# A fused dynamic convolution and MLP: all matmuls of the loop as 64-row tiles on the two row halves, with the transposes inside a second product

## What is computed

```python
# x: (4, 4096, 192); weight_gen: (4, 4096, 8, 7); w_in: (192, 2048); w_out: (2048, 192)
w = exp(weight_gen - max(weight_gen, -1)); w = w / (sum(w, -1) + 1e-9)
out[b,s,h,g] = sum_k w[b,s,h,k] * x_padded[b, s+k, h, g]     # 7 taps, 8 heads of 24 channels
h = out.reshape(16384, 192) @ w_in
y = (s * relu(h)**2 + b) @ w_out                              # (16384, 192), float32
```

## Time and profile before

| | |
|---|---|
| Median of 3 runs | 1248.54 us (1246.58 to 1249.45) |
| The profiled execution | 1249.54 us, span in the trace 1247.7 us |
| Mean granted TensorE clock | 0.991 of full speed |
| PE busy | 96% of the span, 7392 matmuls and as many weight loads |
| DVE, ACT, POOL busy | 80%, 63%, 14% |
| Chain that ended last | PE 73%, ACT 10%, DVE 9%, issue 7% |

### The profile page before, as it was taken

One profiled execution on the slowest core, in us unless ns is written; L12 is line 12 of the kernel. 1 busy time (PEld: TensorE's weight loads), 2 busy tenths in 40 slices (PEclk: granted clock), 3 DMA queues, 4 the chain that ended last, 5 costly groups with the idle time before them and its releaser, 6 DMA issues.

```text
span 1247.7 us, 20056 instructions
## 1 busy us (share of the span) xinstructions
PE 1203.6 (96%) x7392; PEld 1030.6 (83%) x7392; DVE 995.4 (80%) x1162; ACT 780.2 (63%) x844; POOL 172.8 (14%) x97
## 2 busy tenths in 40 slices
PE   3899999999999999999999999999999999999998
PEld 3788888888888888888888888888888888888887
DVE  7887778887778887779887779877788877788853
ACT  3466666666665666665666566666566666666664
POOL 7311011111011110011110111110111110111100
PEclk8899999999999999999999999999999999999999
DMA  5111101111101111101111101111001111011000
GB/s 171 36 49 36 48 16 44 48 48 35 48 13 48 48 48 35 48 13 48 48 48 35 38 22 48 48 39 44 21 39 48 48 35 48 14 47 48 13 0 26
DMA packets 18404, 50.98 MB, mean 41 GB/s; under 512 B 2140, under 2 KB 9563, under 8 KB 18394
## 3 DMA queue, kind: packets, MB, share of 16 engines
q1 hardware_dynamic: 18245, 50.27, 11.9%
q10 hardware_dynamic: 149, 0.59, 0.2%
HBM read 38.27 MB, written 12.58 MB: 41 GB/s over the span
## 4 chain that ended last, share of the span: by engine, by line
PE 73%; ACT 10%; DVE 9%; issue 7%; POOL 1%; DVEq 0%; DMA 0%; ACTq 0%; POOLq 0%
PE op L661 26%; PE hp L637 22%; PE op L663 11%; PE hp L648 11%; ACT r L386 5%; ACT r L390 5%; DVE tap L492 2%; DVE acc L507 2%; PE hp L622 2%; DVE g_hi L534 2%; DVE attn_b L512 1%; PE hp L625 1%; DMA x_in<-in_x 0%; POOL tap_pool L318 0%; POOL acc L327 0%
## 5 line engine op out<-in xcount | busy, mean ns | idle before, releaser
L661 PE MATMUL op<-wo,g_hi 128*128 128x384 f32 x2048 | 608.9, 367 | 2.3 <-DVE g_lo L538 2.3
L663 PE MATMUL op<-wo,g_lo 128*128 128x192 f32 x2048 | 513.4, 251 | 0.0
L386 ACT ACTIVATE r<-hp 128x1024 f32<-128x1024 f32 x256 | 260.1, 1016 | 401.6 <-PE hp L648 397.1
L538 DVE TENSOR_TENSOR g_lo<-r,g_hi 128x1024 fp32r<-128x1024 f32 x256 | 360.0, 1406 | 80.9 <-ACT g_hi L397 76.4
L661 PEld LDWEIGHTS op<-wo,g_hi 128*128 128x128 f32 x2048 | 386.0, 188 | 37.3 <-issue 26.7
L663 PEld LDWEIGHTS op<-wo,g_lo 128*128 128x128 f32 x2048 | 392.7, 192 | 0.0
L637 PE MATMUL hp<-xT,w_hi 128*128 128x512 f32 x1024 | 322.8, 396 | 3.7 <-ACT r L386 1.9
L390 ACT ACTIVATE r<-r 128x1024 f32<-128x1024 f32 x256 | 271.5, 1061 | 7.9
L492 DVE TENSOR_TENSOR tap<-x_in,w_soft 128x768 f32<-128x768 f32 (+1 forms) x192 | 232.8, 1226 | 0.1
L637 PEld LDWEIGHTS hp<-xT,w_hi 128*128 128x128 f32 x1024 | 183.6, 189 | 38.1 <-DVE xT L520 2.2
L637 PE MATMUL hp<-xT,w_lo 128*128 128x512 f32 x512 | 203.4, 397 | 0.0
(11 more groups left out here) (46 smaller groups left out, 418.6 us busy)
## 6 DMA issues: line engine op xcount, KB each, us to landing
x_in<-in_x SPq DMA_DIRECT2D x30, 960.0 KB, 4.8
out<-out_sb SPq DMA_DIRECT2D x31, 384.0 KB, 2.3
w_in<-in_weight_gen SPq DMA_DIRECT2D x32, 112.0 KB, 2.0
wo_raw<-in_moe_w_out SPq DMA_DIRECT2D x4, 384.0 KB, 7.0
w_raw<-in_moe_w_in SPq DMA_DIRECT2D x4, 256.0 KB, 5.4
x_in<-in_x SPq DMA_DIRECT2D x1, 768.0 KB, 6.8
x_in<-in_x ACTq DMA_DIRECT2D x1, 540.0 KB
w_raw<-in_moe_w_in SPq DMA_DIRECT2D x8, 64.0 KB, 4.8
```

The lines of the kernel that those rows point to most:

```text
L386: nc.scalar.activation(r[:, b, :], hp[:, PAIR * b:PAIR * (b + 1), :], ACT.Relu).then_inc(relu_done, 1)
L538: nc.vector.tensor_tensor(g_lo[:, buf, tiles, :], pair, g_hi[:, buf, tiles, :].bitcast(F32), ALU.subtract).then_inc(g_lo_ready, 1)
L661: nc.tensor.matmul(op[:, t, 0:2 * D], g_hi[:, g % 2, j, cols], wo[:, k, :, :].rearrange("p a d -> p (a d)"), start=(k == 0), stop=False)
L663: mm = nc.tensor.matmul(op[:, t, 0:D], g_lo[:, g % 2, j, cols], wo[:, k, 0, :], start=False, stop=(k == FT - 1))
```

## The change

Every matmul with 128 rows in the loop becomes two with 64 rows, one on each half of the partitions. Two matmuls that run side by side write different banks, so each bank is written by one half first and by the other half later; the semaphores `h_bank_left` and `op_bank_left` keep the halves apart. The first product has 18 pairs of matmuls of 512 columns per group; `h_ready` of the even pair comes with pair 15 of them, that of the odd pair with the last. The passes with `xT2` now follow the passes with `xT1` bank by bank, so group 0 needs the copies in the upper partitions (`t_hi_up_ready`, `t_lo_up_ready`) after three pairs. The second product goes by pairs of token tiles outside and hidden tiles j inside, so that pair 2g + 1 is waited for after two units of work. The transposes are 64-row tiles too: 8 for `attn_a` into banks 0 and 1 after a quarter of the second product of group 2, 4 for `attn_b` into banks 2 and 3 after its second quarter. On ScalarE, relu of pair 7 and `hi_of_attn` now stand ahead of the square and the high part of pair 6. `hp` is read for the copies across two banks. In the last step the output is finished in two halves of 2 token tiles instead of 3 and 1.

```diff
+        def block_a():
+            return hp[:, 0:2, 0:STEP * D2].rearrange("p h (t c) -> p t h c", t=STEP)
@@ ScalarE, step
                 for q in range(PAIRS - 1):
                     relu(i, q, first)
+                    if q == PAIRS - 2:
+                        relu(i, PAIRS - 1, first)
+                        if not last:
+                            hi_of_attn(i + 1)
                     square(i, q)
...
-                relu(i, PAIRS - 1, first)
-                if not last:
-                    hi_of_attn(i + 1)
@@ TensorE
+            def transpose_attn_a():
                 for t in range(STEP):
-                    last = nc.tensor.transpose(hp[:, 0, t * P:(t + 1) * P], attn_a[:, t, :], ident[:, :])
+                    for h in range(2):
+                        last = nc.tensor.transpose(hp[:, h, t * D2:(t + 1) * D2], attn_a[rows[h], t, :], ident[rows[h], rows[h]])
...
+            FIRST_BANKS = [((0, True), (2, True), (1, False), (3, False)),
+                           ((1, True), (3, True), (0, False), (2, False))]
...
+                for n, both in enumerate(zip(passes_of(0), passes_of(1))):
+                    if n == 0 and not (first and g == 0):
+                        pe.wait_ge(relu_done, i * PAIRS + 2 * g - 1)
+                    if n == 6 and not (first and g == 0):
+                        pe.wait_ge(relu_done, i * PAIRS + 2 * g)
+                    if n == 3 and g == 0:
+                        pe.wait_ge(t_hi_up_ready, i + 1)
+                        pe.wait_ge(t_lo_up_ready, i + 1)
+                    if n in (12, 15):
+                        pe.wait_ge(h_bank_left, left + n // 3 - 3)
+                    for j, w, xt, start, stop in both:
+                        mm = nc.tensor.matmul(hp[:, j, :], w, xt, start=start, stop=stop)
+                    if n in (5, 11):
+                        mm.then_inc(h_bank_left, 1)
+                    if n in (14, 17):
+                        mm.then_inc(h_ready, 1)
+
+            def second_product(i, g, first=False, last=False, transposes_next=False):
...
+                for n in range(STEP):
+                    transposes_here = transposes_next and n < 2
+                    tiles = ((0, 1), (2, 3), (1, 0), (3, 2))[n]
+                    if n >= PAIR:
+                        pe.wait_ge(op_bank_left, 2 * n_before + n - 1)
+                    for j in range(GROUP):
+                        if n == 0 and j % PAIR == 0:
+                            pe.wait_ge(g_lo_ready, i * PAIRS + 2 * g + j // PAIR + 1)
+                        k = g * GROUP + j
+                        for h, t in enumerate(tiles):
+                            nc.tensor.matmul(op[:, t, 0:2 * D], g_hi[rows[h], g % 2, j, t * P:(t + 1) * P], ...)
+                        if transposes_here and j == GROUP - 1:
+                            if n == 0:
+                                pe.wait_ge(sum_ready, (K - 1) * (i + 2))
+                            pe.wait_ge(relu_done, (i + 1) * PAIRS + n - 1)
+                        for h, t in enumerate(tiles):
+                            mm = nc.tensor.matmul(op[:, t, 0:D], g_lo[rows[h], g % 2, j, t * P:(t + 1) * P], ...)
+                    if n < PAIR:
+                        mm.then_inc(op_bank_left, 1)
+                    if transposes_here and n == 0:
+                        transpose_attn_a()
+                    if transposes_here and n == 1:
+                        transpose_attn_b()
```

More of the change, by code:

```diff
@@ L159, in mix_and_mlp @@
         g_used = sem("g_used")
+        h_bank_left = sem("h_bank_left")
+        op_bank_left = sem("op_bank_left")
         out_sums_ready = sem("out_sums_ready")
@@ L225, in store_last @@
             def store_last():
-                first = (STEPS - 1) * STEP * row
-                for n, (a, b) in enumerate(((0, EARLY), (EARLY, STEP))):
+                last_rows = out_rows[:, (STEPS - 1) * STEP * row:STEPS * STEP * row].rearrange("p (t d) -> p t d", t=STEP)
+                for n in range(2):
                     sp.wait_ge(last_output_ready, n + 1)
-                    sp.dma_start(out_rows[:, first + a * row:first + b * row],
-                                 out_sb[:, a:b, :].rearrange("p t d -> p (t d)")).then_inc(last_stored, FETCH)
+                    sp.dma_start(last_rows[:, n * PAIR:(n + 1) * PAIR, :], out_sb[:, n * PAIR:(n + 1) * PAIR, :]).then_inc(last_stored, FETCH)
             load_w(0)
@@ L544, in last_output @@
                 dve.wait_ge(out_stored, FETCH * (STEPS - 1))
-                for n, tiles in enumerate((slice(0, EARLY), slice(EARLY, STEP))):
+                for n in range(2):
                     if n == 0:
@@ L549, in last_output @@
                         dve.wait_ge(g_used, NG * STEPS)
-                    m = tiles.stop - tiles.start
-                    nc.vector.scalar_tensor_tensor(out=out_sums[:, tiles, 0:D], in0=op[:, tiles, 0:D], scalar=s_col[:, 0:1],
-                                                   in1=bias[:, :].unsqueeze(1).to_broadcast([P, m, D]),
+                    nc.vector.scalar_tensor_tensor(out=out_sums[:, n * PAIR:(n + 1) * PAIR, 0:D], in0=op[:, n * PAIR:(n + 1) * PAIR, 0:D], scalar=s_col[:, 0:1],
+                                                   in1=bias[:, :].unsqueeze(1).to_broadcast([P, STEP // 2, D]),
                                                    op0=ALU.mult, op1=ALU.add).then_inc(last_part_ready, 1)
                     dve.wait_ge(last_part_ready, n + 1)
-                    nc.vector.scalar_tensor_tensor(out=out_sb[:, tiles, :], in0=op[:, tiles, D:2 * D], scalar=s_col[:, 0:1],
-                                                   in1=out_sums[:, tiles, 0:D], op0=ALU.mult,
+                    nc.vector.scalar_tensor_tensor(out=out_sb[:, n * PAIR:(n + 1) * PAIR, :], in0=op[:, n * PAIR:(n + 1) * PAIR, D:2 * D], scalar=s_col[:, 0:1],
+                                                   in1=out_sums[:, n * PAIR:(n + 1) * PAIR, 0:D], op0=ALU.mult,
                                                    op1=ALU.add).then_inc(last_output_ready, 1)
@@ L624, in transpose_attn @@
                 for u in range(STEP // 2):
-                    last = nc.tensor.transpose(hp[:, 1, u * P:(u + 1) * P],
-                                               attn_b[:, 2 * u:2 * u + 2, :].rearrange("p t d -> p (t d)"), ident[:, :])
+                    for h in range(2):
+                        last = nc.tensor.transpose(hp[:, 2 + h, u * D2:(u + 1) * D2],
+                                                   attn_b[rows[h], 2 * u:2 * u + 2, :].rearrange("p t d -> p (t d)"),
+                                                   ident[rows[h], rows[h]])
@@ L627, in transpose_attn @@
                 last.then_inc(t_ready, 1)
+            FIRST_BANKS = [((0, True), (2, True), (1, False), (3, False)),
+                           ((1, True), (3, True), (0, False), (2, False))]
             def first_product(i, g, first=False):
[L630 to L666, removed]
+                def passes_of(h):
+                    for j, own in FIRST_BANKS[h]:
+                        f = slice((g * GROUP + j) * P, (g * GROUP + j + 1) * P)
+                        f2 = slice((g * PAIR + j // 2) * P, (g * PAIR + j // 2 + 1) * P)
+                        some = [(w1_hi[rows[h], f], xT1[rows[h], 0, :]), (w1_hi[rows[h], f], xT1[rows[h], 1, :]),
+                                (w1_lo[rows[h], f], xT1[rows[h], 0, :])]
+                        if own:
+                            some += [(w2_hi[rows[h], f2], xT2[rows[h], 0, :]), (w2_hi[rows[h], f2], xT2[rows[h], 1, :]),
+                                     (w2_lo[rows[h], f2], xT2[rows[h], 0, :])]
+                        for n, (w, xt) in enumerate(some):
+                            yield j, w, xt, own and n == 0, not own and n == len(some) - 1
@@ new lines, in first_product @@
+                left = 2 * (i * NG + g)
+                for n, both in enumerate(zip(passes_of(0), passes_of(1))):
[14 more added lines that the diff above has]
+                        mm.then_inc(h_ready, 1)
@@ new lines, in second_product @@
+            def second_product(i, g, first=False, last=False, transposes_next=False):
+                n_before = i * NG + g
+                if first:
+                    pe.wait_ge(wo_lo_ready, g + 1)
+                if not (first and g == 0):
+                    pe.wait_ge(g_used, n_before)
+                for n in range(STEP):
[8 more added lines that the diff above has]
+                        for h, t in enumerate(tiles):
+                            nc.tensor.matmul(op[:, t, 0:2 * D], g_hi[rows[h], g % 2, j, t * P:(t + 1) * P],
+                                             wo[rows[h], k, :, :].rearrange("p a d -> p (a d)"),
+                                             start=(k == 0 and n < PAIR), stop=False)
+                        if transposes_here and j == GROUP - 1:
[3 more added lines that the diff above has]
+                        for h, t in enumerate(tiles):
```

(12 more changed lines are left out.)

17 lines of the change are left out of this document (10 added, 7 removed).

## The result

| | before | after |
|---|---|---|
| Median (lowest to highest) | 1247.66 us (1246.58 to 1249.45) | 1273.87 us (1271.76 to 1274.46) |
| Profiled execution, span | 1249.54, 1247.7 us | 1271.76, 1269.8 us |
| Mean granted clock | 0.991 | 0.980 |
| Matmuls | 7392 | 13216 |

The ratio is 1.0206 [1.0187, 1.0224]: the change makes the kernel 26 us slower, where 22 us less was forecast. 1273.87 is near rival 1's lower price, 1276.

A forecast was written before the change was run, and what follows sets the result against it. TensorE's own stream was taken to set the time, busy 37.17 of 37.70 us per step. From 1249.54, 30 steps by -0.8, first step +1.0, last +0.7 gave 1227 profiled, 1226 us median; range 1205 to 1365.

The forecast's parts named there:

- rival 1: GpSimd's request precedes VectorE's cast of pair 1: TensorE waits 2.68 us, 1276 us total, 1360 with clock falls; chance 0.38.
- Where it hangs: Whether GpSimd's addition or VectorE's cast of pair 1 asks first; sum put GpSimd 0.13 us ahead, forecast took the cast.
- the forecast's order: VectorE's cast of pair 1 goes ahead of GpSimd's first addition; TensorE then waits 1.03 us for pair 1.
- What goes: On TensorE, shape changes (0.36 per group, 1.44 us per step) and the 0.5 hole before transposes vanish: 1.9 to 2.0.
- The doubled matmuls: TensorE's 64-row matmuls cost nothing extra per column: 0.232 per pair, 0.287 per unit; six transposes keep 0.66 per step.
- rival 3: TensorE's sequencer limits the unit to 0.40: +5.7 us per step, 1430 us; chance 0.06.
- rival 4: TensorE's units get a little slower, 0.30 each, and eat the gain: 37.7 per step, no change; chance 0.07.
- Pair 7: Second product of group 3: TensorE waits 0.18 us for g_lo of pair 7.
- Pair 1: Second product of group 0: TensorE waits 1.03 us for g_lo of pair 1, or 2.68 if GpSimd asks first.
- The clock's price: A 2.68 wait every step may bring 5.7 us at half clock each time, 2.8 lost: 1276 becomes 1360 us.
- The two ends: First step +1.0 us and last step +0.7 us, outside the 30 steps in between.
- 12.89: VectorE's way from g_lo of pair 6 to g_lo of pair 1, taken as 12.89 us of unbroken work.

The follow-up runs named there:

- experiment 2: Changed kernel, but GpSimd starts its additions only when g_lo of pair 0 of the next step is done; 1212.87 us, ratio 0.9721.
- experiment 1: Changed kernel, but GpSimd starts its additions only when g_lo of pair 1 of the next step is done; 1193.88 us, ratio 0.957.
- experiment 3: Changed kernel, but each second product waits for its odd pair after eight units again, GpSimd left as it is; 1209.05 us, ratio 0.9685.
- experiment 5: Changed kernel with the odd pair awaited after eight units and GpSimd adding after g_lo of pair 1; 1179.99 us, ratio 0.946.
- experiment 7: As experiment 5, but relu of pair 7 and hi_of_attn go back behind the high part of pair 6 on ScalarE; 1218.49 us, ratio 0.9766.

## Why the prediction was wrong

**The step that failed is "Where it hangs".** In the kernel before, GpSimd asks 0.70 us behind the start of the cast. The working put its request 0.13 ahead of the cast; the changed kernel has it 0.19 ahead. The prediction then set the sum aside, "TensorE's side has more terms that can only grow", and took the other case. That sentence held an asymmetry that no row showed, and the terms shrank. In the step shown above T, the start of the second product of group 2, is 640.87; its rows:
```profile
640.87 0.34 PE L693 MATMUL op<-wo,g_hi 64*128 64x384 f32 x2
...
647.64 1.23 DVE L546 TENSOR_TENSOR g_lo<-r,g_hi 128x1024 fp32r<-128x1024 f32 x1 [0.77 <-ACT g_hi L403]
...
649.79 1.03 ACT L392 ACTIVATE r<-hp 128x1024 f32<-128x1024 f32 x1 [0.95 <-PE hp L671]
```
On GpSimd's side, T to the next step is 5.17 instead of 5.25, from there to relu 0 it is 3.75 as taken, and from relu 0 to GpSimd 6.92 instead of 6.99: T + 15.84 instead of 15.99. On VectorE's side, `g_lo` of pair 6 starts at T + 6.77 instead of 6.86 and the cast follows 9.26 later as taken: T + 16.03 instead of 16.12. So the sum was right to 0.06 us. What followed from the order was nearly right on both sides: with the requests in the forecast's order (experiment 2) a step is 36.53 (36.9 forecast) and the time 1212.87 us (1226 forecast); with GpSimd first it is 38.15 (38.56 in rival 1). Experiments 1 and 3 show the two parts of the wait, GpSimd's blocks and TensorE's early need, each taken away alone.

**What goes** was right. No 0.36 per group is left in the changed kernel, and the hole of 0.53 ahead of the transposes is gone; a wait of 0.16 of the weight loads is left (experiment 5's list of waits). Experiment 5 makes the gain visible where nothing waits: 37.70 - 35.49 = 2.2 per step.

**The doubled matmuls** cost nothing per column, as taken: pairs 0.231, units 0.287 (15 from 672.15 to 676.45), with eight instructions in a unit. This closes rivals 3 and 4. (Rival 3's price had a slip: 0.40 - 0.287 is 0.113 and not 0.12, so 5.2 per step and not 5.7.) The transposes came out just under their lower bound of 0.33: eight occupy 0.21 and four 0.08 to 0.09, twelve 0.30 instead of 0.66. What is left of the block from T to the next step, 5.17 - 4.59 - 0.30 = 0.28, is the wait for the sums and small restarts.

**Pair 7** waits less than the 0.18 computed: the third unit of that second product starts at 650.79, 0.04 late.

**Pair 1** waits 2.45, computed 2.68: the first block is 1.65 and not 1.7, the second 1.5 and not 1.65. Step by step at full clock: 38.56 less 0.08 (transposes' block), 0.07 (pairs), 0.08 (group 3) and 0.23 (pair 1) is 38.10; 38.15 is measured.

**The clock's price** was the badly sized term of rival 1. The same idle stretch in every step dropped it in 9 of 28 steps, not in none or all, and a fall cost 39.73 - 38.15 = 1.58, not 2.8: the fall shown above lasted some 3.4 us (from about 663.7 to 667.1), where the first step of the earlier trace rows had stood at 0.50 for over 5.7. Idle stretches of 0.68, 0.74 and 0.98 in every step (experiments 2, 3 and 7) brought no fall. What makes one stretch of 2.31 bring a fall and the next not, no run shows.

**The two ends** were taken at +1.7 together; by the account above everything outside the 28 steps gave back 4.9 us, since the first of GpSimd's additions came 2.15 earlier, the second step and the last but one ran in the forecast's order, and the last waits only 0.27 and 0.95 (1.8 had been taken).

**Chances.** Rival 1 was given 0.38 against 0.44 for the forecast. The sum that was written down spoke for rival 1, and the blind margin, 0.13 against 27 slots and waits, did not justify turning it over: the two should at best have been even, with the time put by the sum.

The Trainium skill (SBUF — State Buffer, section "Who interferes with whom") states "Issue order, not op shape, decides who blocks." Experiment 2, the second step and the last but one of the changed kernel agree, with 0.49 to 0.68 us of idle on TensorE in one order and 2.31 in the other.

**The two steps with the other order** can be read in part. They are written out on VectorE, while the 28 between run inside its loop (`dve.Fori`). In the 28, VectorE idles 0.23 ahead of its first tap; in the two it doesn't. The first line is from a step of the loop, the second from the second step:
```profile
652.29 0.96 DVE L499 TENSOR_TENSOR acc<-x_in,w_soft 128x768 f32<-128x768 f32 x1 [0.23 <-DVE w_soft L479]
...
75.53 0.96 DVE L499 TENSOR_TENSOR acc<-x_in,w_soft 128x768 f32<-128x768 f32 x1
```
From `g_lo` of pair 6 to the cast it is 9.06 in the second step (71.08 to 80.14) and 9.26 in the loop. That makes 0.20 of the shift of 0.26 between the requests; the rest is GpSimd's side, 0.06 later. In the last step but one it is 9.07, which is all of the shift of 0.19. The kernel before has the same 28 idle stretches, so its 12.89 contained one. Why the loop brings it is not shown.

**Left open.** The price of a change of tile shape was tested on the transposes only, so whether all of the 0.36 per group belongs to it is open. What the tile shape alone would bring, with the transposes and ScalarE's order in their old places, was not tried.

## What to carry to other kernels

When a sum puts two requests for a shared resource a tenth of a microsecond apart, write down both outcomes and follow the sum; better still, force the order by a wait, as the one line on GpSimd does here for 80 us. An edit that speeds up the bounding engine moves every place where it asks for another engine's work: check for each how far before its use the work is finished, and keep the late user (eight units instead of two) unless the new order needs it. Work of an engine with slack (GpSimd, busy 13%) goes behind the last item on the critical way, not ahead of it.

## What the runs showed that was not expected

- An idle stretch of TensorE of 2.31 us, the same to 0.01 in each of 28 steps, is followed by a fall of the granted clock in 9 of them, every third or fourth, at 1.58 us each.
- Two 64-row matmuls side by side with their own loads keep the rate of one 128-row matmul at 384 and 192 columns (0.287 per unit), with twice the instructions.
- Eight 64 x 64 transposes do the work of four of 128 x 128 in half their time: 0.21 us against four slots of 0.10 to 0.11.
- GpSimd's first addition lasts 1.99 to 2.09 us when it asks ahead of the cast (changed kernel, experiment 3) and 2.23 to 2.50 when VectorE is at work as it asks (experiments 2 and 1). In the kernel before, where the cast has just ended, it is 1.85.
- VectorE idles 0.23 us ahead of its first tap in the 28 steps of its loop and not in the second step and the last but one; here that is most or all of the shift in the order of the two requests.
